# Scalars and alpha loaded by DMA into their columns, with the order of the start changed on three engines

## What is computed

```python
qn = q / (norm(q, axis=1) + 1e-06)          # q, k: 6016 x 256, norms of the 256 columns
kn = k / (norm(k, axis=1) + 1e-06)
s = kn.T @ qn / tau                         # 256 x 256
a = exp(s - s.max(-1));  a /= a.sum(-1) + 1e-09
x = v @ a                                   # 6016 x 256
g = moe_s * relu(x @ moe_w_in) ** 2 + moe_b # w_in: 256 x 2048
x = g @ moe_w_out                           # w_out: 2048 x 256
h = x @ moe2_w_in
out = (max(h, 0) + alpha * min(h, 0)) @ moe2_w_out   # alpha: 2048 numbers
```

## Time and profile before

| | |
|---|---|
| time, median of 3 executions | 1034.34 us (1034.32 to 1034.74) |
| the profiled execution | 1034.81 us, of which the span 1033.0 us |
| TensorE busy | 1025.7 us, 99% of the span |
| VectorE busy | 846.0 us, 82% |
| ScalarE busy | 617.4 us, 60% |
| GpSimd busy | 60.0 us, 6% |
| granted TensorE clock | full in all slices shown |

### The profile page before, as it was taken

The page is one execution under the profiler, slowest core; times in us unless marked ns, Lnnn a source line. Parts: engine busy times, 40 slices in busy tenths (PEclk is TensorE's granted clock), DMA queues, the critical chain, the costliest instruction groups (busy, mean ns, idle before and its releaser), DMA issues.

```text
span 1033.0 us, 13283 instructions
## 1 busy us (share of the span) xinstructions
PE 1025.7 (99%) x4579; PEld 858.0 (83%) x4579; DVE 846.0 (82%) x1287; ACT 617.4 (60%) x1031; POOL 60.0 (6%) x88
## 2 busy tenths in 40 slices
PE   9999999999999999999999999999999999999997
PEld 8768888888888888888998888888888888888997
DVE  6888888889788888788998988777778777877875
ACT  5577776666566566566676665455545455544553
POOL 1023100000000000000561000000000000000000
PEclk9999999999999999999999999999999999999999
DMA  9953303302402211300641246004104203200201
GB/s 357 264 82 66 63 1 123 62 1 82 102 1 82 82 19 39 123 1 31 226 162 49 90 161 178 6 0 153 31 1 143 41 1 125 42 0 1 41 1 36
DMA packets 130851, 79.26 MB, mean 77 GB/s; under 512 B 98450, under 2 KB 107232, under 8 KB 130784
## 3 DMA queue, kind: packets, MB, share of 16 engines
q1 hardware_dynamic: 125536, 71.63, 23.1%
q0 software_dynamic: 4096, 6.44, 2.9%
q10 hardware_dynamic: 1152, 0.34, 0.1%
HBM read 50.54 MB, written 27.72 MB: 76 GB/s over the span
## 4 chain that ended last, share of the span: by engine, by line
PE 95%; DVE 2%; DMA 2%; ACT 0%; issue 0%; SPq 0%; POOL 0%; DVEq 0%; ACTq 0%; POOLq 0%
PE acc L493 16%; PE acc L494 16%; PE acc L495 16%; PE hab L493 8%; PE hab L494 8%; PE hab L495 8%; PE hcd L493 6%; PE hcd L494 6%; PE hcd L495 6%; DMA qk_raw<-in_q_dram 2%; DVE sq_sum L1132 1%; PE acc L609 1%; PE acc L587 0%; PE hab L617 0%; SPq L337 0%
## 5 line engine op out<-in xcount | busy, mean ns | idle before, releaser
L775 ACT ACTIVATE g_hi<-cb 128x512 fp32r<-128x512 f32 (+1 forms) x384 | 233.3, 619 | 155.8 <-DVE cb L1012 84.1
L493 PE MATMUL acc<-g_hi,wo_hi 128*128 128x512 f32 (+1 forms) x766 | 295.1, 385 | 0.0
L495 PE MATMUL acc<-g_hi,wo_lo 128*128 128x512 f32 (+1 forms) x766 | 295.1, 385 | 0.0
L494 PE MATMUL acc<-g_lo,wo_hi 128*128 128x512 f32 (+1 forms) x766 | 295.0, 385 | 0.0
L1018 DVE TENSOR_TENSOR g_lo<-cb,g_hi 128x512 fp32r<-128x512 f32 (+1 forms) x384 | 246.0, 681 | 41.1 <-ACT g_hi L775 39.2
L495 PEld LDWEIGHTS acc<-g_hi,wo_lo 128*128 128x128 f32 x766 | 143.8, 188 | 27.0
L493 PEld LDWEIGHTS acc<-g_hi,wo_hi 128*128 128x128 f32 x766 | 143.8, 188 | 26.9 <-DVE g_lo L1018 0.2
L494 PEld LDWEIGHTS acc<-g_lo,wo_hi 128*128 128x128 f32 x766 | 143.8, 188 | 26.7
L1012 DVE SCALAR_TENSOR_TENSOR cb<-cb,alph 128x512 f32<-128x512 f32 (+1 forms) x192 | 142.3, 741 | 20.6 <-ACT cb L745 14.5
L493 PE MATMUL hab<-x_hi,ws_hi 128*128 128x512 f32 (+1 forms) x384 | 149.2, 388 | 0.0
L494 PE MATMUL hab<-x_lo,ws_hi 128*128 128x512 f32 (+1 forms) x384 | 148.0, 385 | 0.0
(11 more groups left out here) (130 smaller groups left out, 969.0 us busy)
## 6 DMA issues: line engine op xcount, KB each, us to landing
x_dram<-x_hi SPq DMA_DIRECT2D x35, 256.0 KB, 2.2
x_dram<-x_lo SPq DMA_DIRECT2D x35, 256.0 KB, 2.6
x_hi<-x_dram SPq DMA_DIRECT2D x35, 256.0 KB, 4.8
x_lo<-x_dram SPq DMA_DIRECT2D x35, 256.0 KB, 5.0
out_dram<-y_sq SPq DMA_DIRECT2D x40, 128.0 KB, 2.9
v_raw<-in_v_dram SPq DMA_DIRECT2D x36, 128.0 KB, 3.3
qk_raw<-in_k_dram SPq DMA_DIRECT2D x8, 512.0 KB, 11.4
qk_raw<-in_q_dram SPq DMA_DIRECT2D x8, 512.0 KB, 12.3
```

The source lines that it names most:

```text
L493: pe.matmul(dst, w_hi, m_hi, start=start, stop=False, skip_group_check=True)
L494: pe.matmul(dst, w_hi, m_lo, start=False, stop=False, skip_group_check=True)
L495: return pe.matmul(dst, w_lo, m_hi, start=False, stop=stop, skip_group_check=True)
L775: sc.activation(g_hi[:, blk, 0:w], cb[:, blk, 0:w], ACT.Copy).then_inc(g_hi_done[blk], 1)
```

## The change

Three things are changed.

1. **Scalars and alpha.** The matmul and the transpose on TensorE (L626, L627) and the copies on VectorE are gone. GpSimd loads each scalar straight to a column of 128 partitions, at the place where it loaded them to one partition. Alpha comes in 16 loads of one column each (128 pieces of 4 bytes), after the two loads of `colsum`. VectorE computes `rtau` from the loaded scalar before it waits for the square roots, and `sign` in step 10 behind a wait for the 16 loads.
2. **TensorE's order.** Two rows of half 1 stand ahead of the column sums; five rows of it stand between them and the spread norms, where there were six, and five in place of six behind.
3. **VectorE's and ScalarE's order.** On VectorE `turn_v(0, 0, 1)` moves behind `largest(0)`, and `largest(1)` moves ahead of `x_low(0, 1)` and `turn_v(0, 1, b)`. On ScalarE `x_high(0, 1)` moves behind the first copy of the transposed half, and `a_copy(1)` ahead of `w0_high(0)` and `x_high(0, 2)`.

```diff
-            pool.dma_start(scal_row[0:1, n:n + 1], x.rearrange("(a n) -> a n", a=1)).then_inc(small_loaded, 16)
-            pool.dma_start(alpha_row[0:NF, :], moe2_alpha.rearrange("(f p) -> f p", p=P)).then_inc(small_loaded, 16)
+            pool.dma_start(scal[:, n:n + 1], x.rearrange("(a n) -> a n", a=1).broadcast_to((P, 1))).then_inc(scal_loaded, 16)
...
+            for f in range(NF):
+                pool.dma_start(alph[:, f:f + 1], moe2_alpha[f * P:(f + 1) * P].rearrange("(p a) -> p a", a=1)).then_inc(alpha_loaded, 16)
...
-                if i == LATE:
-                    pe.wait_ge(consts_ready, 5)
-                    pe.wait_ge(small_loaded, 64)
-                    pe.matmul(scal_ps[:, 0:3], ones[0:1, :], scal_row[0:1, 0:3], start=True, stop=True)
-                    pe.transpose(alpha_ps, alpha_row[0:NF, :], ident[0:NF, 0:NF]).then_inc(cols_ready, 1)
...
+            scores(late, 1, range(2))
             pe.wait_ge(squares_added, ADDED[-1] + 1)
...
-            scores(late, 1)
-            scores(late + 1, 1, range(CHUNK // 2))
+            scores(late, 1, range(2, CHUNK))
+            scores(late + 1, 1, range(CHUNK - 1))
             pe.wait_ge(diag_ready, 1)
...
-            scores(late + 1, 1, range(CHUNK // 2, CHUNK))
+            scores(late + 1, 1, range(CHUNK - 1, CHUNK))
...
-                sc.wait_ge(v_turned, 2 * CB * run + (2, 2, 4)[min(i, 2)])
+                sc.wait_ge(v_turned, 2 * CB * run + (1, 2, 4)[min(i, 2)])
...
             x_high(0, 0)
-            x_high(0, 1)
...
             soften(0)
             a_copy(0)
-            x_high(0, 2)
+            x_high(0, 1)
             soften(1)
             w1_copy(0)
+            a_copy(1)
             w0_high(0)
-            a_copy(1)
+            x_high(0, 2)
...
+                if n == STEPS + 2:
+                    ve.wait_ge(alpha_loaded, 16 * NF)
+                    link(ve.tensor_scalar(sign[:], alph[:], 1.0, -2.0, ALU.is_gt, ALU.mult))
+                    link(ve.tensor_scalar(sign[:], sign[:], 1.0, None, ALU.add))
...
+            ve.wait_ge(scal_loaded, 16 * 3)
+            link(ve.reciprocal(rtau, scal[:, 0:1]))
             ve.wait_ge(root_ready, 1)
...
-            ve.wait_ge(cols_ready, 1)
-            link(ve.tensor_copy(scal, scal_ps[:, 0:3]))
-            link(ve.reciprocal(rtau, scal[:, 0:1]))
             link(ve.tensor_scalar(rk, rnorm[:, 2:4], rtau, None, ALU.mult))
-            for b in range(CB):
-                turn_v(0, 0, b)
+            turn_v(0, 0, 0)
...
             largest(0)
+            turn_v(0, 0, 1)
             x_low(0, 0, x_hi_done, x_split)
             inverse_sum(0)
+            largest(1)
             x_low(0, 1, x_hi_done, x_split)
-            link(ve.tensor_copy(alph[:], alpha_ps))
-            link(ve.tensor_scalar(sign[:], alph[:], 1.0, -2.0, ALU.is_gt, ALU.mult))
-            link(ve.tensor_scalar(sign[:], sign[:], 1.0, None, ALU.add))
             for b in range(CB):
                 turn_v(0, 1, b)
-            largest(1)
             x_sums(0)
```

More of the change, by code:

```diff
@@ L164, in build @@
         rq_diag = at("rq_diag", 171 * K, [CB, P], F32)
-        alpha_row = at("alpha_row", 172 * K, [P], F32)
-        scal_row = at("scal_row", 172 * K + 512, [4], F32)
         root = col[:, 4:8]
@@ L197, in build @@
         cols_ps = acc[1][:, 0, 0:16]
-        scal_ps = h_d[:, 16:20]
-        alpha_ps = h_d[:, 32:32 + NF]
         rq_ps = acc[1][:, 1, 0:C]
         a_t_ps = [acc[1][:, m, 0:C].rearrange("p (b c) -> p b c", b=CB) for m in range(CB)]
-        small_loaded = sem("small_loaded")
+        scal_loaded = sem("scal_loaded")
+        alpha_loaded = sem("alpha_loaded")
         qk_loaded = [sem(f"qk_loaded{i}") for i in range(RAW)]
@@ L855, in _ @@
             sc.wait_ge(consts_ready, 5)
-            sc.wait_ge(cols_ready, 2)
+            sc.wait_ge(cols_ready, 1)
             sc.activation(root, cols_ps[:, 0:4], ACT.Sqrt, bias=tiny).then_inc(root_ready, 1)
```

## The result

| | before | changed |
|---|---|---|
| time, median (8 runs of each) | 1034.91 us (1034.32 to 1036.47) | 1038.48 us (1037.37 to 1039.17) |
| ratio, 95% interval | 1 | 1.0032 (1.0024 to 1.0041) |
| the profiled execution | 1034.81 us, span 1033.0 us | 1039.17 us, span 1037.4 us |
| TensorE busy | 1025.7 us | 1027.1 us |
| VectorE busy | 846.0 us | 846.4 us |

What follows compares the result with a forecast made beforehand. TensorE was read as waiting only 1.4 us in all, 0.14% of the time. Terms 0.1 (S2 later) and 0.05 (scalar loads) gave about +0.15 us, 1034.5 against the median 1034.34; range 1033.4 to 1035.7.

Steps and rivals of the forecast that it cites:

- Loads of the scalars: Three loads on GpSimd while chunks arrive: 96 packets of 12 ns, 0.07 us an engine, taken as 0.05 us.
- three loads of 128 pieces from one address: Rival: scalar loads hold up q and k chunks, measurably slower from 86 ns a piece; over 2.07 us got chance 0.05.
- Ahead of them: Two score rows before the column sums: their 0.89 us fits TensorE's 0.92 us idle time and costs nothing.
- The sum from the column sums on: From column sums through S2's low matmul: S2 comes 0.1 us later than before, then nothing waits.
- The new wait on VectorE: Ahead of the second half's logits, VectorE stands still about 1.07 us for the last score row, other work queued behind.
- TensorE's 0.9 us: After the second transpose, TensorE itself reaches the last blocks 0.9 us earlier, at 52.6 in place of 53.51.
- Loads of alpha: 16 issues on GpSimd end at 123.4, needed about 167.5 in step 10: 40 us of cover, no cost.

Runs made afterwards that it cites:

- order_only: The changed kernel with scalars and alpha loaded to one partition and 16 rows and spread by TensorE as before, new order kept: 1035.09 us, ratio 0.9999.
- behind_chunks: The changed kernel with its three scalar loads issued only when the last chunk of q and k has landed: 1035.34 us, ratio 1.0005.
- loads_only: The kernel before with the new loads of the scalars and alpha alone, the engines' order as before: 1036.85 us, ratio 1.0016.
- many_addresses: The changed kernel with each of the three early loads reading 128 different numbers of alpha, not one scalar 128 times: 1036.16 us, ratio 1.0011.
- low_first: order_only with one transpose of the second tile and `x_low(0, 1)` moved ahead of the second half's logits on VectorE: 1034.40 us, ratio 0.9995.
- sign_later: The kernel before with VectorE's scalar and alpha copies and inverse of tau ahead of its wait for the roots, `sign` in step 10: 1034.04 us, ratio 0.9993.
- six_broadcasts: The changed kernel with three more one-address loads of tau at the start, into columns that nothing reads: 1039.59 us, ratio 1.0053.
- warm_in_gap: The changed kernel with ten unused 128x128 matmuls on TensorE behind chunk 0's scores: 1037.43 us, ratio 1.0025.
- rows_back: The changed kernel with the two score rows of half 1 put back behind the column sums: 1038.15 us, ratio 1.0037.
- one_broadcast: The changed kernel with only tau's load at the start, those of moe_s and moe_b behind colsum's loads: 1036.26 us, ratio 1.0013.

## Why the prediction was wrong

**The step that failed is the term "Loads of the scalars".** It took 0.05 us, from 96 packets of 12 ns, and the sentence "the column sums stay at 41.26, since the squares' chain on VectorE is not changed" rests on it. Number and duration of the packets were as forecast, 96 of 12 ns. But they were not the cost: the squares ended 2.06 later, as the DMA engines were mostly without a packet (share 0.17 to 0.40 from 3 to 7 us, 0.93 to 1.08 before). The mechanism was among the rivals, and a cost of over 2.07 us by it was given 0.05: "three loads of 128 pieces from one address ... in front of and between the chunks". Its price there, "each ns that a piece takes an engine costs 24 ns", let the cost show only as a longer packet, and its evidence was a row of pieces at different addresses. The prediction says so itself; it was the only evidence against the rival and did not bear on it. With no row of the case for reads of one address, both ends should have stayed open. In the rival's own terms the price was 2.06 us / 24 = 86 ns a piece, at its threshold. The range's upper end has a further 0.2 us for the loads. No run shows that term; in its place the runs showed squares that end 2.06 us later.

**"Ahead of them ... Cost nothing; what hides them is the wait for VectorE, and without it they would cost 0.89."** Right as a condition and wrong in what became of it. In order_only and behind_chunks the sums stay at 41.33 and 40.68, so the wait covers the rows, if with nothing to spare. In the changed kernel's profile the wait was gone: to the late chunks came a second cost that stands in no step, half pace until 13.8 instead of 6.3. Together TensorE was 1.84 behind the squares. Of when TensorE leaves the half pace of its start the prediction says nothing. It differs between profiles for no reason that the runs show (4.6 in loads_only, 6.3 before, 10.1 in many_addresses; 4.0 to 13.9 over all 13), so this part of the loss is in part chance. Worked out from loads_only, 0.89 of that are the rows and 1.15 the longer stretch at half pace, less 0.26 of cover.

**The sum from the column sums on was right.** Forecast 19.4 (+0.1), measured 19.45 (+0.14); order_only has 19.46. With the column sums at 41.33 the second logits were forecast at 49.05 and came at 49.07, the wait ahead of them 1.07 and 1.01, A12's low matmul 58.28 and 58.38 (wait 1.2 and 1.26), S2 60.7 and 60.79. The new wait on VectorE took TensorE's 0.9 us, and low_first shows it: with that work moved, the stretch is 0.84 shorter.

**Loads of alpha.** Right as far as the profile goes: no wait of TensorE stands in step 10 of the changed kernel. The 0.34 us more behind S2 are not explained. They lie within what that stretch varies: 972.35 us in sign_later and 972.77 in low_first, neither of which has the loads of alpha. A slip of about 0.13 between 110 and 140 us, where alpha's loads are issued and land, was not separated from that.

**Shares of the 3.6 us.** In time, against the kernel before: the order alone +0.2 to +0.3, within noise; the loads alone +2.05; both +3.6. What is left over, about 1.3, is by the profiles the rows without cover and the longer half pace; no run separates the two in time, and the intervals of loads_only and the changed kernel touch. That one address is the cause of most of the hold-up is shown by many_addresses; that it is the place in the stream, by behind_chunks; that it grows with the number of loads, by one and six. Why reads of one address bring the engines' share down to 0.17 is not settled: the profile has no row for where a read waits. Nor was it tried how few reads of one address are harmless, or whether the queue that issues them matters.

## What to carry to other kernels

A load that spreads one number over 128 partitions reads that one address 128 times. While the chunks streamed in, each such load put the end of the squares 0.7 to 1.1 us later here, though its packets look free (96 for three loads, 12 ns each). Behind the stream the three cost nothing measurable (1035.34 us, ratio 1.0005), and neither did one number spread by TensorE (order_only, 1035.09, ratio 0.9999). So in a like case try one of these two. A cost that the profile of before doesn't show for this very kind of access has no upper bound from a neighbouring row, and a rival that names it deserves a chance that says so. And work moved into another engine's wait is free only as long as nothing makes that engine faster or its own start later: check both ends of the cover. Last, a profile is one execution: what varies between executions, as the moment of TensorE's full pace does here (4.0 to 13.9 us), can't be put down to the change from it alone.

## What the runs showed of the hardware

- **Three loads that read one address 128 times each, and the DMA engines.** In the changed kernel they bring the mean share of the 16 engines to 0.37, 0.40, 0.17 and 0.38 from 3 to 7 us (1.08, 0.95, 0.93 and 1.01 before), and what is moved from 1206 KB to 404. With six (six_broadcasts) there is a second hold-up, with 0.11 from 9 to 10 us. Loads of the same size from 128 addresses (many_addresses) leave the share at 0.58 and 0.80 from 3 to 5 us and at 1.07 and 1.02 from 5 to 7. The three loads land 4.2, 5.4 and 6.4 us after their issue; those from 128 addresses land after 3.5 (median), and the same three behind the stream (behind_chunks) after 3.8 to 4.4.
- **TensorE starts at half pace in all 13 profiled executions.** The first 12 records of 128x128 take 2.93 us in each, 0.24 a record, and in the changed kernel the first score records start 0.43 apart; at full pace it is 0.12 (warm_in_gap) and 0.215. The first clock record of the trace begins where the pace changes: at 6.31 us before, at 6.63 in order_only, 10.07 in many_addresses and 13.87 in the changed kernel; the earliest is 3.98, in sign_later. The clock column reads 1.00 ahead of that record as well, so the pace of equal instructions is the surer reading there.
- **The clock fell at gaps of 2.50 to 2.89 us.** In loads_only it goes from 1.00 to 0.50 at 7.96 us, by the end of a gap of 2.86 us, and is back at 1.00 at 11.38. In six_broadcasts it stands at 0.50 from 7.46 to 10.87, with a gap of 2.89 us that ends at 7.80, and in rows_back from 8.29 to 11.71, behind a gap of 2.50 us that ends at 7.82. In one_broadcast a gap of 1.30 us brought no fall: the clock reads 1.00 in every window from 7 to 16 us, and the 158 records behind the gap take 34.37 us, all at full pace.
